# Moving two groups of a rational activation's denominator from a DMA accumulate to VectorE and GpSimd, with shorter lags

## The reference

```python
w = exp(weight_gen - max(weight_gen)); w = w / (sum(w) + 1e-9)
conv[b, s, h, :] = sum_k w[b, s, h, k] * x_pad[b, s + k, h, :]     # 6 zero rows ahead of each sequence
h = conv.reshape(16384, 192) @ w_in                                 # 192 x 2048
P = a[0] + a[1]*h + a[2]*h**2 + a[3]*h**3
Q = 1 + abs(b[0])*abs(h) + abs(b[1])*h**2
out = (P / (Q + 1e-6)) @ w_out                                      # 2048 x 192
```

## Time and profile before

| | |
|---|---|
| median of 3 runs | 1421.39 us (1420.86 to 1421.90) |
| the profiled execution's own time | 1420.86 us |
| its span from first to last instruction | 1419.1 us |
| PE busy (matmuls) | 1307.0 us, 92% |
| ACT busy | 1270.7 us, 90% |
| DVE busy | 1214.8 us, 86% |
| POOL busy | 1036.6 us, 73% |
| granted TensorE clock, mean | 0.992 |

### The profile page before, as it was taken

One profiled execution on the slowest core, in us unless ns is written; L12 is line 12 of the kernel. 1 busy time (PEld: TensorE's weight loads), 2 busy tenths in 40 slices (PEclk: granted clock), 3 DMA queues, 4 the chain that ended last, 5 costly groups with the idle time before them and its releaser, 6 DMA issues.

```text
span 1419.1 us, 19150 instructions
## 1 busy us (share of the span) xinstructions
PE 1307.0 (92%) x6912; PEld 1178.2 (83%) x6912; DVE 1214.8 (86%) x872; ACT 1270.7 (90%) x1030; POOL 1036.6 (73%) x672
## 2 busy tenths in 40 slices
PE   0279999999999999999999999999999999999997
PEld 0268898888898888889888888988888888888897
DVE  2988898899889889989888998988988898898775
ACT  1278999999999999999999999999999999999995
POOL 1878787787878778878777887877788787787210
PEclk9889999999999999999999999999999999999999
DMA  2534444534544544454454354445345445533432
GB/s 89 144 90 110 103 117 114 128 85 107 131 94 114 125 117 88 115 120 105 109 131 107 87 126 108 117 109 131 87 102 131 97 117 120 119 83 81 100 68 67
DMA packets 35486, 152.21 MB, mean 107 GB/s; under 512 B 3992, under 2 KB 10260, under 8 KB 35472
## 3 DMA queue, kind: packets, MB, share of 16 engines
q0 software_dynamic: 18432, 100.67, 34.9%
q1 hardware_dynamic: 16752, 51.36, 10.5%
q10 hardware_dynamic: 288, 0.00, 0.0%
HBM read 38.78 MB, written 12.58 MB: 36 GB/s over the span
## 4 chain that ended last, share of the span: by engine, by line
PE 62%; ACT 25%; issue 7%; DVE 4%; DMA 2%; SPq 0%; ACTq 0%; DVEq 0%
PE ops L690 33%; PE hps L680 28%; ACT num L479 7%; ACT beta L474 6%; ACT den L452 6%; ACT den L471 4%; DMA xwin<-in_x 2%; ACT out_sb L446 2%; PE hps L665 1%; DVE gate L543 1%; DVE conv L554 1%; ACT den L455 1%; DVE gate L605 0%; DVE wi_lo L561 0%; DVE num L621 0%
## 5 line engine op out<-in xcount | busy, mean ns | idle before, releaser
L690 PE MATMUL ops<-wo,gate 128*128 128x192 f32 x4096 | 702.2, 327 | 41.7 <-ACT out_sb L446 35.8
L690 PEld LDWEIGHTS ops<-wo,gate 128*128 128x128 f32 x4096 | 676.0, 191 | 69.8 <-issue 48.5
L621 DVE TENSOR_TENSOR num<-num,hps 128x1536 f32<-128x1536 f32 (+1 forms) x192 | 301.6, 1571 | 153.4 <-ACT num L479 153.4
L327 POOL TENSOR_TENSOR conv<-conv,prod 128x768 f32<-128x768 f32 (+2 forms) x192 | 395.2, 2058 | 15.0
L605 DVE SCALAR_TENSOR_TENSOR gate<-num,coef,den 128x1536 f32<-128x1536 f32 (+1 forms) x192 | 375.0, 1953 | 2.6 <-issue 1.6
L323 POOL TENSOR_TENSOR prod<-xwin,taps 128x768 f32<-128x768 f32 (+2 forms) x192 | 336.7, 1754 | 3.4
L624 DVE SCALAR_TENSOR_TENSOR num<-num,coef,hps 128x1536 f32<-128x1536 f32 (+1 forms) x192 | 314.2, 1637 | 6.8
L346 POOL DMA_DIRECT2D den<-beta x128 | 112.7, 881 | 265.8 <-ACT beta L474 260.3
L479 ACT ACTIVATE num<-hps,coef 128x1536 f32<-128x1536 f32 (+1 forms) x192 | 287.8, 1499 | 0.0
L452 ACT ACTIVATE den<-den,one_eps 128x1536 f32<-128x1536 f32 (+1 forms) x192 | 277.8, 1447 | 0.0
L471 ACT ACTIVATE den<-hps,absb 128x1536 f32<-128x1536 f32 x128 | 196.6, 1536 | 77.1 <-PE hps L680 70.5
(11 more groups left out here) (52 smaller groups left out, 766.5 us busy)
## 6 DMA issues: line engine op xcount, KB each, us to landing
den<-beta POOLq DMA_DIRECT2D x128, 768.0 KB, 5.6
xwin<-in_x SPq DMA_DIRECT2D x30, 960.0 KB
out<-out_sb SPq DMA_DIRECT2D x32, 384.0 KB, 3.8
taps_raw<-in_weight_gen SPq DMA_DIRECT2D x32, 112.0 KB, 3.9
wo<-in_moe_w_out SPq DMA_DIRECT2D x1, 1536.0 KB, 13.6
num<-in_moe_w_in SPq DMA_DIRECT2D x2, 512.0 KB, 6.6
num<-in_moe_w_in SPq DMA_DIRECT2D x4, 256.0 KB, 7.9
xwin<-in_x SPq DMA_DIRECT2D x1, 768.0 KB
```

Source lines behind the costliest of these rows:

```text
L327: pool.tensor_tensor(conv[parity][:, cols], conv[parity][:, cols], prod[k % 2][:, cols], ALU.add).then_inc(conv_steps, 1)
L621: dve.tensor_tensor(slot(num, g), slot(num, g), h_of(q), ALU.mult).then_inc(num2_ready, 1)
L690: last = pe.matmul(ops[:, j // 2, (j % 2) * D:(j % 2 + 1) * D], gate[:, g % GATE_RING, n * COLS + j * P:n * COLS + (j + 1) * P], wo[:, c, ...
```

## The change

Group 0 and group 3 leave DMA_GROUPS and are finished by a beta on POOL and a product on DVE, as group 1 is. Group 4 goes from DVE's product to POOL's. Groups 2 and 5 keep the DMA. All lags are shorter by one: INVERT_LAG 1, GATE_LAG 2, LAG 3; the rings of num and den have 3 slots, that of beta 2. The scratch tiles dprod of DVE's opening convolution, which lay in gate's ring, get their own memory. DVE's three root steps move behind the convolution of tile 1.

```diff
-INVERT_LAG = 2
-GATE_LAG = 3
-LAG = 4
-RING = 4
+INVERT_LAG = 1
+GATE_LAG = 2
+LAG = 3
+RING = 3
 GATE_RING = 3
-BETA_RING = 3
-POOL_GROUPS = ()
-DMA_GROUPS = (0, 2, 3, 5)
+POOL_GROUPS = (4,)
+DMA_GROUPS = (2, 5)
...
+        dprod = [sb(f"dprod{n}", [P, ROW]) for n in range(3)]
...
-        beta = sb("beta", [P, BETA_RING, GW])
+        beta = sb("beta", [P, 2, GW])
         gate = sb("gate", [P, GATE_RING, GW])
-        dprod = [gate[:, n, 0:ROW] for n in range(3)]
...
# POOL, group(): and the same two lines in ACT's tile(), ahead of the Square
-                if not first or q >= BETA_RING:
-                    wait_q(pool, t if q >= BETA_RING else t - 1, (q - BETA_RING) % GROUPS)
+                if not first or q >= 2:
+                    wait_q(pool, t if q >= 2 else t - 1, (q - 2) % GROUPS)
...
# DVE, opening
             pre_conv(0)
-            dve.wait_ge(root_guess, 1)
-            dve.reciprocal(root[:, 1:2], root[:, 0:1]).then_inc(root_inverse, 1)
...
-            dve.tensor_scalar(root[:, 2:3], root[:, 2:3], 0.5, None, ALU.mult).then_inc(root_ready, 1)
             wi_lo_half(0)
...
             pre_conv(1)
             dve.wait_ge(small_loaded, 2 * 16)
+            dve.wait_ge(root_guess, 1)
+            dve.reciprocal(root[:, 1:2], root[:, 0:1]).then_inc(root_inverse, 1)
...
+            dve.tensor_scalar(root[:, 2:3], root[:, 2:3], 0.5, None, ALU.mult).then_inc(root_ready, 1)
```

More of the change, by code:

```diff
@@ L471, in tile @@
                         act.activation(slot(den, g), h_of(q), ACT.Abs, scale=absb[:, 0:1]).then_inc(abs_ready, 1)
-                        if not first or q >= BETA_RING:
-                            wait_q(act, t if q >= BETA_RING else t - 1, (q - BETA_RING) % GROUPS)
+                        if not first or q >= 2:
+                            wait_q(act, t if q >= 2 else t - 1, (q - 2) % GROUPS)
                         act.activation(slot(beta, g), h_of(q), ACT.Square, scale=root[:, 2:3]).then_inc(square_ready, 1)
@@ L597, in _ @@
             dve.wait_ge(small_loaded, 2 * 16)
+            dve.wait_ge(root_guess, 1)
+            dve.reciprocal(root[:, 1:2], root[:, 0:1]).then_inc(root_inverse, 1)
+            dve.wait_ge(root_inverse, 1)
+            dve.scalar_tensor_tensor(root[:, 2:3], root[:, 1:2], absb[:, 1:2], root[:, 0:1], ALU.mult,
+                                     ALU.add).then_inc(root_twice, 1)
+            dve.wait_ge(root_twice, 1)
+            dve.tensor_scalar(root[:, 2:3], root[:, 2:3], 0.5, None, ALU.mult).then_inc(root_ready, 1)
             def gate_of(i, g, ring_full):
```

## The result

The changed kernel takes 1492.9 us (1492.22 to 1493.83) against 1421.64 for the kernel before, measured beside it: ratio 1.0501, 95% interval 1.0483 to 1.0520.

What follows compares the result with a forecast made beforehand. It took POOL and DVE operations that cannot overlap to bound the tile: POOL 32.3 plus DVE 14.6 is 46.9, taken as 46.7 us. 1420.86 + 150 - 2.3 - 4 gave 1565 us, range 1505 to 1649.

Steps and rivals of the forecast that it cites:

- The bound and its cause: POOL and DVE's two-SBUF-input operations exclude each other and set the tile at 46.7 us, in place of PE's 40.54.
- the size of a turn: Non-overlapping POOL and DVE operations per tile, each at its clean duration: POOL 32.3 us, DVE 14.6, sum 46.9.
- the floor of 44.7: Lowest tile of the main case: 46.9 us less at most 2.2 for overlap at hand-overs between POOL and DVE.
- the tile laid out by hand: One tile scheduled with the estimated durations; group 0's beta came back 46.7 us later, POOL never waiting for an Abs.
- its 49.5: Upper tile of the main case: POOL's queue of 34.9 us, issues and gaps included, plus every DVE operation at full length.
- The step from tiles to time: Tiles 0 to 29 add +150 us, tiles 30 and 31 -2.3, the end -4, on 1420.86: 1565.
- The range: Whole kernel at 1505 to 1649 us, from a main-case tile of 44.7 to 49.5 us, given 0.83.
- the short lags: Lags and rings shortened by one: waits on earlier groups already later in DVE's and POOL's order, so no cost.
- the landing: Accumulating DMA's data in place 5.6 us after issue, about 1.4 and 1.5 us after ACT's Ln is reached; costed at nothing.
- A: PE stays the bound because POOL's and DVE's operations hide in idle time: tile 40.54 us, time 1380; chance 0.05.
- D: POOL's beta is slow in itself, not blocked: tile 46 to 50 us, inside the range; no chance of its own.
- C: Engines' orders wait on each other beyond the queue, and PE's clock falls: tile 50.7 us, time 1685; chance 0.10.

Runs made afterwards that it cites:

- e4: Separate small kernel, 12 operations of each shape on POOL alone, DVE alone, then both: adds 21.1 us, gates 20.8, together 39.3.
- e6: Changed kernel, DVE's den*beta product one place earlier and reading h in PSUM instead of beta: 1380.7 us; the same move without PSUM 1474.0.
- e11: Changed kernel with the long lags and rings back (INVERT_LAG 2, GATE_LAG 3, LAG 4, RING 4): 1462.1 us, 1.029 of the kernel before.
- e13: Changed kernel with beta's ring 3 in place of 2: 1491.8 us, 1.050 of the kernel before.
- e12: Kernel before with the shorter lags and rings of num and den, plus group 4's product on POOL: 1468.4 us, 1.033 of the kernel before.
- e3: Changed kernel with group 4's product back on DVE (POOL_GROUPS empty): 1575.2 us, 1.108 of the kernel before.
- e8: Kernel before with short lags (1, 2, 3), RING 4, DMA_GROUPS 2 and 5, POOL_GROUPS empty: 1540.5 us, 1.083 of the kernel before.
- e10: Changed kernel with groups 0 and 3 back on the DMA, group 4's product still on POOL: 1468.8 us, 1.034 of the kernel before.
- e1: Kernel before with only the shorter lags and rings of num and den (1, 2, 3, RING 3): 1375.1 us, 0.968 of the kernel before.
- e2: Kernel before with only the new groups (POOL_GROUPS 4, DMA_GROUPS 2 and 5), long lags: 1460.6 us, 1.028 of the kernel before.

## Why the forecast failed, point by point

**The bound and its cause: right.** POOL and DVE's operations with two SBUF inputs take turns, so the tile is POOL's queue with DVE's turns in it. POOL is busy over 98% of the 20 tiles (874.3 of 886.95 us) and waits for nobody, the wait for out_sb is gone, ACT is busy 36.8 us (36 forecast), DVE's large gates last 2.67 (above 2.5 forecast), the large beta 1.63 (near 1.8). PE idles 3.6 us a tile where 6 were forecast, since the tile is shorter. e4 and e6 show the cause directly.

**The step that failed: the size of a turn, on both sides.** The prediction charged DVE 14.6 us and POOL 32.3, each operation at the whole length of a clean record, summed them to 46.9 and took 46.7. In the changed kernel, from one subtraction to the next (702.51 to 746.85), DVE's nine turns, each from the end of POOL's operation to the end of DVE's, are 1.62 for each large gate, 1.09 for a small one, 1.62 for a large product and 1.08 for the small one, 13.0 in all. POOL's own operations, measured in the same way from the end before, are 30.1, and its two DMA issues, which the sum of 46.9 left out, 1.3. So DVE's part was 1.6 too high, POOL's 2.2 too high, and 1.3 was missing: 44.4.
- DVE's large product was put at 1.30 x 1.5 = 1.95. The 1.30 holds 0.2 that isn't turn: 1.08 x 1.5 = 1.62. Two products, 0.66; the small one, charged at the whole 1.30, 0.22. POOL's large beta likewise, 1.62 for 1.79, 0.34 together.
- A gate's clean duration (1.72, 1.27) was charged whole; its turn is 1.62 and 1.09. Six gates, 0.76.
- An add was charged at 1.83. All six stand straight behind a turn of DVE in the changed kernel and take 1.68 to 1.72 each, 0.8 together; the six products are 0.6 less, mostly for the same reason.
- The first multiplication was charged at 1.85, read where it stood behind a DMA issue. With group 0 off the DMA it takes 1.54, as do POOL's other products; only those behind an issue take 1.8. 0.3.

The turns stood in the rows of the kernel before: its small product ended 1.08 us after POOL's (708.25 against 707.17), its gate 1.61 after the add. The prediction saw the overlap, 0.12 at each hand-over, and put it into the floor of 44.7 only. How the tile laid out by hand came to 46.7, with the issues and gaps that its 49.5 contains, can't be followed from what is written. The 19 gaps of 0.07 in that 49.5 are wrong as well: a gap (0.08) stands behind POOL's products of the convolution, none behind its adds, and in e4 twelve adds take 21.1 us, 1.76 each, for records of 1.80.

**The step from tiles to time held, partly by luck.** By the prediction's formula 30 x 2.64 - 6.3 is +72.9, and +71.6 were measured. But the opening lost 3.2, which was costed at nothing: 1.7 is the product of group 0 in front of DVE's max of the taps, for which POOL's first subtraction waits, and most of the rest lies in DVE's opening convolution, where it meets POOL's first betas. And the stretch from the subtraction of tile 28 on, nearly two tiles with a convolution and two without, gained 5.5 where the formula has 1.5. The two misses nearly cancel.

**The range** was too narrow at the low end. Its floor of 44.7 took off the most that the hand-overs could give, but started from a product, a beta and a multiplication that were too long, and let no other error add to it; the steady tile is 44.35.

**Costed at nothing, rightly:** the root steps, dprod and beta's ring (e11, e13). **Costed at nothing, wrongly:** the short lags, which with the new groups cost 31 us (e11), by shifting where DVE's turns fall, as far as the rows tell. **Costed at nothing, not settled:** the landing. The prediction had it land 1.4 and 1.5 us after ACT came for it; ACT waits 6.8 us a tile, 3.4 for each. In e12 such a wait sets the pace, in the changed kernel POOL, which never waits, does.

**Rivals.** A needed less than 5.6 us of blocking beside a queue of 34.9; the queue was 31.4 with its issues, but there were 13.0 us of turns. D falls by e4. C, mutual waiting, was given 0.10 as an addition to the queue. In the change POOL waits for nobody, so it has no place, but e3, e8, e10 and e12 are of its kind, and the count of turns missed them: by 126 us in e3, by 79 to 94 in e10.

## What to carry to other kernels

Before work is moved to an engine with room, look whether its operations can run beside those of its neighbour: put the two engines' single instructions side by side, and read what ends when, since waiting inside the engine counts as busy. Add up what can't overlap, by turns taken (end to end), not by durations, and only then compare with the bound. Such a sum holds for one queue and one order: with several queues close to full, one product moved or the lags changed by one was worth 19 to 93 us here, in either direction, so try the parts of a change one at a time. Here the lags alone were the better kernel, 1375.1 us.

## What the hardware showed that was not expected

- The turn of a DVE operation with two SBUF inputs beside POOL is 1.08 to 1.09 us for 1024 columns and 1.62 for 1536, in proportion to the columns, while its record alone is 1.22 to 1.27 and 1.72 to 1.75.
- The two don't always alternate: beside betas of 1536 columns, twelve gates were through in 26.9 us, while the betas took 37.6; beside adds both ended together, after 39.3 and 37.8.
- The accumulating DMA lands in 5.6 us when it is issued 2.8 us behind a 960 KB load, in 6.0 to 6.2 at 2.3 behind, in about 7 at 1.3 and in 8.8 to 10.3 at 0.3 to 0.5 (before, e1, e12, e10).
- Issuing a DMA on POOL takes no turn: DVE's gate runs beside the issue, and only the operation behind it is held (e2, 711.08 to 714.15).
- The same instructions in the same order ran at two rhythms, 42.3 and 47.6 us a tile, within one execution (e3).
